# A three-stage kernel on one Trainium2 core: output columns split at row 64, small steps moved between engines

## The reference, cut to what matters

```python
scores = q @ k.T / 8; causal mask; a = exp(scores - rowmax)
a /= a.sum(-1) + 1e-9;  local = a @ v
q_p = where(q > 0, q, exp(q) - 1) + 1                  # "phi"
mem_out = (q_p @ M_prev) / (q_p @ z_prev + 1e-6)
x = g * mem_out + (1 - g) * local                      # g = sigmoid(beta) per head
x = act(x @ w_in) @ w_out                              # 512 -> 2048 -> 512
out = capacity-limited top-1 experts over x, 8 experts 512 -> 1024 -> 512
```

## Time and profile before

| | |
|---|---|
| runs | 307.69 us median (306.95 to 309.27, 3 runs) |
| the profiled execution | 307.44 us, its span 305.3 us |
| busy | PE 98%, DVE 71%, ACT 50%, POOL 45% |
| granted TensorE clock | 1.000, full speed throughout |
| prologue / rounds 1 to 7 / round 8 | 0 to 14.43 / 14.43 to 98.77 / 98.77 to 111.71 us |

### The profile page before, as it was taken

The page is one execution under the profiler, slowest core; times in us unless marked ns, Lnnn a source line. Parts: engine busy times, 40 slices in busy tenths (PEclk is TensorE's granted clock), DMA queues, the critical chain, the costliest instruction groups (busy, mean ns, idle before and its releaser), DMA issues.

```text
span 305.3 us, 7256 instructions
## 1 busy us (share of the span) xinstructions
PE 297.8 (98%) x2821; PEld 247.5 (81%) x2821; DVE 217.4 (71%) x583; ACT 151.4 (50%) x332; POOL 136.4 (45%) x154
## 2 busy tenths in 40 slices
PE   7999999999999999999999999999999999999993
PEld 6666676676666988887999998999989898996863
DVE  3999998999978367897885557955785559880520
ACT  1796866867766244655551444345344546501110
POOL 4878997998998300373782003003312334020031
PEclk9999999999999999999999999999999999999999
DMA  8999798861537700000000407751015019349980
GB/s 164 158 207 228 191 203 174 192 172 46 166 68 206 228 5 0 2 2 0 2 0 2 77 2 287 266 90 30 0 20 93 7 18 384 150 124 392 354 320 9
DMA packets 75047, 38.48 MB, mean 126 GB/s; under 512 B 66008, under 2 KB 66016, under 8 KB 73988
## 3 DMA queue, kind: packets, MB, share of 16 engines
q1 hardware_dynamic: 72340, 36.74, 45.8%
q10 hardware_dynamic: 2416, 0.59, 1.0%
q0 software_dynamic: 256, 0.67, 0.6%
HBM read 32.66 MB, written 5.39 MB: 125 GB/s over the span
## 4 chain that ended last, share of the span: by engine, by line
PE 94%; POOL 2%; DVE 1%; issue 1%; ACT 0%; POOLq 0%
PE bank_a L1841 17%; PE bank_b L1841 17%; PE bank_out L1798 6%; PE bank_a L1697 4%; PE bank_b L1901 4%; PE bank_pt L1901 4%; PE bank_pt L1749 4%; PE bank_a L1775 3%; PE bank_out L1795 2%; PE bank_a L2080 2%; PE bank_out L1874 2%; PE bank_b L2080 2%; PE bank_b L1692 2%; PE bank_out L2189 2%; PE bank_out L1786 2%; PE bank_a L2090 2%
## 5 line engine op out<-in xcount | busy, mean ns | idle before, releaser
L720 POOL TENSOR_SCALAR prob<-prob,rl,gate_loc 128x512 f32<-128x512 f32 (+3 forms) x64 | 41.5, 662 | 11.0 <-DVE rl L1230 11.0
L1841 PE MATMUL bank_a<-x_hi,win_hi 128*128 128x288 f32 x128 | 39.3, 307 | 0.0
L1841 PE MATMUL bank_b<-x_hi,win_hi 128*128 128x288 f32 x128 | 38.2, 298 | 0.0
L1841 PE MATMUL bank_b<-x_lo,win_hi 128*128 128x288 f32 x128 | 38.0, 297 | 0.0
L1841 PE MATMUL bank_b<-x_hi,win_lo 128*128 128x288 f32 x128 | 38.0, 297 | 0.0
L1841 PE MATMUL bank_a<-x_hi,win_lo 128*128 128x288 f32 x128 | 38.0, 297 | 0.0
L1841 PE MATMUL bank_a<-x_lo,win_hi 128*128 128x288 f32 x128 | 37.9, 296 | 0.0
L972 ACT ACTIVATE g_raw<-bank_a,biases 128x576 f32<-128x576 f32 x16 | 11.9, 742 | 49.5 <-DVE sq L1310 49.5
L909 ACT ACTIVATE prob<-prob,negmax 128x512 f32<-128x512 f32 (+3 forms) x64 | 35.0, 549 | 0.3 <-DVE negmax L1180 0.3
L804 POOL TENSOR_TENSOR w_lo<-w_sb,w_hi 128x512 fp32r<-128x512 f32 x8 | 11.4, 1426 | 48.2 <-ACT w_hi L1015 48.2
L749 POOL TENSOR_TENSOR x_lo<-xT,x_hi 128x1152 fp32r<-128x1152 f32 x4 | 10.6, 2662 | 48.6 <-ACT x_hi L922 48.6
(11 more groups left out here) (322 smaller groups left out, 792.2 us busy)
## 6 DMA issues: line engine op xcount, KB each, us to landing
w_sb<-in_moe_w_dram SPq DMA_DIRECT2D x6, 2048.0 KB, 12.0
win_raw<-in_moe_w_in_dram SPq DMA_DIRECT2D x4, 1024.0 KB, 5.6
wout<-in_moe_w_out_dram SPq DMA_DIRECT2D x4, 1024.0 KB, 6.1
win_raw<-in_moe_w_in_dram SPq DMA_DIRECT2D x1, 4096.0 KB, 13.6
out_dram<-zero_row SPq DMA_DIRECT2D x8, 288.0 KB
x_d<-x_rows SPq DMA_DIRECT2D x32, 72.0 KB, 2.1
v_sb<-in_v_dram SPq DMA_DIRECT2D x16, 128.0 KB, 2.5
qn<-in_q_dram SPq DMA_DIRECT2D x24, 72.0 KB, 5.4
```

The lines of the kernel that those rows point to most:

```text
L720: pool.tensor_scalar(prob[u][:, h, :], prob[u][:, h, :], rl[:, c:c + 1], gate_loc[:, 2 * j + h:2 * j + h + 1], ALU.mult, ALU.mult).then_in ...
L1841: last = pe.matmul(h_bank(d)[:, t, :], w[:, m, f:f + P], x[c % 2][:, m, :], start=(m == 0 and n == 0), stop=(m == KT - 1 and n == 2))
```

## The change

1. The tokens now begin at column 448 of `bank_out`: 64 in the first bank, 512 in the second. The memory term is cut the same way, a tile of 64 first, then four of 128. All products of a pair with v stand in one function, six per head with 192, 320, 448, 64, 64 and 512 columns, in place of nine.
2. TensorE's order behind `turn_prob(j, 6)` becomes `add_memory(j)`, `memory(r)`, `values(j)`; `values` waits for copies 2, 5 and 6 before its first product.
3. ScalarE adds the 1e-9 (`row_sums`, behind `exp_s(r, 2)` and `below_zero(r + 1)`, and behind `exp_s(r, 4)`); VectorE keeps the reciprocal alone.
4. Pair 1's q and k are loaded in blocks and turned by VectorE, behind `row_max(0, 4)`; TensorE's ten transposes and VectorE's three copies go. Loads of pair 3 wait for these buffers.
5. From round 2 on, `turn_k(r + 1)` moves from the start of VectorE's round to behind `row_max(r, 4)`; in round 0 `row_factor(0, 1)` stands ahead of `scale_memory(0)`.
6. `few_hidden` goes behind f = 4.

```diff
+        X_AT = NFULL * P - TAIL
+        def mem_tile(t):
+            at = max(0, TAIL + (t - 1) * P)
+            return at, P if t else TAIL
...
-                if n > 3:
+                if n > 2:
                     sp.wait_ge(s_qe, n - 1)
...
-            load_tiles(sp, q_rows[1], q3[2:4, :, :], s_qrow[1])
+            load_blocks(sp, qn[1], q3[2:4, :, :], s_q[1])
...
+            def row_sums(i, part):
+                cols = slice(0, 4) if part == 0 else slice(4, 9)
+                act.wait_ge(s_exp, 5 * i + (2 if part == 0 else 5))
+                act.activation(rl[:, cols], rsum[:, cols], ACT.Identity, bias=biases[:, 2:3]).then_inc(s_eps, 1)
...
             def row_factor(i, part):
                 cols = slice(0, 4) if part == 0 else slice(4, 9)
-                dve.wait_ge(s_exp, 5 * i + (2 if part == 0 else 5))
-                dve.tensor_scalar(rl[:, cols], rsum[:, cols], 1e-9, None, ALU.add).then_inc(s_rl, 1)
-                dve.wait_ge(s_rl, 4 * i + 2 * part + 1)
+                dve.wait_ge(s_eps, 2 * i + part + 1)
                 dve.reciprocal(rl[:, cols], rl[:, cols]).then_inc(s_rl, 1)
...
-            copy_q(1)
-            copy_k(1)
             dve.wait_ge(s_tail, 3)
             row_max(0, 4)
+            turn_q(1)
+            turn_k(1)
+            row_factor(0, 1)
             scale_memory(0)
...
-                    turn_k(r + 1)
-                if r == 1:
-                    row_factor(0, 1)
...
                     row_max(r, 4)
+                if 1 < r < NPAIR - 1:
+                    turn_k(r + 1)
...
-                for c in reversed(range(NFULL)):
-                    times_v(j, c, False)
-            def last_values(j):
                 copied(j, 6)
-                for c in range(NT):
-                    last = times_v(j, c, True)
+                for c, q0, q1 in ((3, 3 * P, S), (2, 2 * P, S), (1, P, S), (NFULL, NFULL * P, S), (0, 0, TAIL), (0, TAIL, S)):
+                    w = P if c < NFULL else TAIL
+                    for h in range(2):
+                        last = pe.matmul(bank_out[D * h:D * h + D, X_AT + q0:X_AT + q1], v_sb[j % 2][0:w, c, h, :],
+                                         probT[0:w, h, c * KSTEP + q0:c * KSTEP + q1], start=False, stop=(c == 0))
...
+                if r == 0:
+                    memory(0)
                 if r > 0:
-                    values(j)
+                    add_memory(j)
                 if 0 < r < NPAIR:
                     memory(r)
-                if r == 0:
-                    turn_k(1)
-                    memory(0)
                 if r > 0:
-                    last_values(j)
+                    values(j)
...
-                if f == 5:
+                if f == 4:
                     few_hidden()
```

More of the change, by code:

```diff
@@ L125, in build_program @@
         mem = [sb(f"mem{p}", [P, NT, 2, D], F32)[0] for p in range(2)]
-        q_rows = [sb(f"q_rows{p}", [P, NT, 2, D], F32, at=xT_at + 4 * NT * P * p)[0] for p in range(2)]
-        k_rows = [sb(f"k_rows{p}", [P, NT, 2, D], F32, at=xT_at + 4 * NT * P * (2 + p))[0] for p in range(2)]
-        assert 16 * NT * P <= 4 * NPAIR * S
+        q_rows, _, _ = sb("q_rows", [P, NT, 2, D], F32, at=xT_at)
+        k_rows, _, _ = sb("k_rows", [P, NT, 2, D], F32, at=xT_at + 4 * NT * P)
+        assert 8 * NT * P <= 4 * NPAIR * S
         maskw, _, _ = sb("maskw", [P, NFULL * P], F32)
@@ L286, in build_program @@
         s_k = [sem(f"s_k{p}") for p in range(2)]
-        s_qrow = [sem(f"s_qrow{p}") for p in range(2)]
-        s_krow = [sem(f"s_krow{p}") for p in range(2)]
+        s_qrow = sem("s_qrow")
+        s_krow = sem("s_krow")
         s_qt = sem("s_qt")
@@ L307, in build_program @@
         s_exp = sem("s_exp")
+        s_eps = sem("s_eps")
         s_rl = sem("s_rl")
@@ L1708, in turn_rows, with turn_q, turn_k @@
                 return last
[L1710 to L1726, removed]
+            def turn_q():
+                pe.wait_ge(s_qrow, 48)
+                turn_rows(bank_b, q_rows, range(NT)).then_inc(s_qt, 1)
+            def turn_k():
+                pe.wait_ge(s_krow, 48)
+                turn_rows(bank_out, k_rows, range(NT)).then_inc(s_kt, 1)
             def spread_beta():
@@ L1742, in turn_prob @@
                 if j == 0 and g == 0:
-                    pe.wait_ge(s_qe, 2)
+                    pe.wait_ge(s_zc, 1)
+                if j == 0 and g == 1:
+                    pe.wait_ge(s_gates, 1)
                 copied(j - (g < 2), (g - 2) % NPT)
@@ L1772, in memory @@
                 for t in range(NT):
+                    at, w = mem_tile(t)
                     for h in range(2):
                         part = slice(D * h, D * h + D)
-                        last = pe.matmul(mem_bank(i)[0:rows[t], t, h, :], qpT[i % 2][part, t * P:t * P + rows[t]], mz[part, i, :],
-                                         start=True, stop=True)
+                        last = pe.matmul(mem_bank(i)[0:w, t, h, :], qpT[i % 2][part, at:at + w], mz[part, i, :], start=True, stop=True)
                 last.then_inc(s_nm, 1)
@@ L1784, in add_memory @@
                 for t in range(NT):
[L1785 to L1795, removed]
-                                         probT[0:w, h, c * KSTEP + NFULL * P:c * KSTEP + S], start=False, stop=(c == NFULL))
-                    else:
-                        last = pe.matmul(bank_t[part, c * P:NFULL * P], v_sb[j % 2][:, c, h, :],
-                                         probT[:, h, c * KSTEP + c * P:c * KSTEP + NFULL * P], start=False, stop=(c == 0))
-                return last
+                    at, w = mem_tile(t)
+                    pe.matmul(bank_out[:, X_AT + at:X_AT + at + w], mem[j % 2][0:w, t, :, :].rearrange("p h d -> p (h d)"),
+                              ident[0:w, 0:w], is_transpose=True, start=(t < 2), stop=False)
             def values(j):
                 pe.wait_ge(s_v[j % 2], 48 * (j // 2 + 1))
-                add_memory(j)
                 copied(j, 2)
                 copied(j, 5)
-                for c in reversed(range(NFULL)):
-                    times_v(j, c, False)
-            def last_values(j):
                 copied(j, 6)
-                for c in range(NT):
-                    last = times_v(j, c, True)
+                for c, q0, q1 in ((3, 3 * P, S), (2, 2 * P, S), (1, P, S), (NFULL, NFULL * P, S), (0, 0, TAIL), (0, TAIL, S)):
[3 more added lines that the diff above has]
+                                         probT[0:w, h, c * KSTEP + q0:c * KSTEP + q1], start=False, stop=(c == 0))
                 last.then_inc(s_pv, 1)
@@ L1964, in keep_running @@
                 for i in range(n):
-                    at = (NT + i % 2) * P
+                    at = S + i % 2 * P
                     pe.transpose(bank_out[:, at:at + P], ident[:, :], ident[:, :])
             keep_running(18)
-            turn_k(0)
-            turn_q(0)
+            turn_k()
+            turn_q()
             spread_beta()
```

76 lines of the change are left out of this document (39 added, 37 removed).

## The result

The changed kernel takes 310.62 us (median of 7 runs, 309.85 to 311.2) against 307.69 us (7 runs, 306.81 to 309.27): ratio 1.0094, 95% interval 1.0074 to 1.0113. On a second chip it took 310.47 us (4 runs) against 308.21 us: 1.0074 (1.0049 to 1.0099). The forecast was 310.0 us and its sum +2.4 us; measured are +2.9 and +2.3 us. The profiled execution took 310.62 us, 3.2 us more than the one before. Its span is 308.8 us instead of 305.3, 3.5 us more; what lies outside the span went from 2.1 to 1.8 us.

A forecast was written before the change was run, and what follows sets the result against it. TensorE was taken to bound the kernel, holding 94% of the chain that ended last. Terms +1.0, +1.4, +0.2, 0, 0 and -0.2 sum to +2.4 us on 307.44; forecast 310.0 us, range 306.8 to 312.0.

The forecast's parts named there:

- The output split: TensorE's six products a head for nine: one more shape change, +0.10 us a round, +0.27 in round 8, sum +1.0.
- Rival A: The output split pays: new shape changes cost nothing, -2.4 us in place of +1.0, 306.6 us; chance 0.13.
- Memory ahead of values in round 1: TensorE in round 1 waits at memory(1) for phi(1), behind ScalarE's sum and the reciprocal: +1.4 us, bounds +0.9 and +1.6.
- Rival D: Round 1 doesn't wait, because VectorE's and ScalarE's work shifts with TensorE's: 308.6 us; chance 0.12.
- Values behind copy 6: First values product waits for copy 6: no wait in rounds 2 to 5 and 7, +0.2 us in round 6.
- The 1e-9 on ScalarE: Addition off VectorE, where GpSimd's subtraction held it and copy 6 would come late by 0.4 us; by itself worth 0.
- Rival B: Reciprocal or ScalarE's sum late, so values wait for copy 6: 0.4 us in six rounds, 312.4 us; chance 0.12.
- Pair 1 by VectorE: Prologue and round 1: earlier memory(0) and GpSimd factors against a later row maximum; sum 0, bounds -0.2 and +0.5 us.
- Rival C: Pair 1's blocks land late, at 14.6 us instead of under 13.4: +1.2 us, 311.2 us; chance 0.08.
- Left tokens: Last stage: few_hidden a step forward removes TensorE's wait for g_fewT, -0.2 us, bounds -0.6 and 0.

The follow-up runs named there:

- e3: Changed kernel with memory tiles in order 1, 2, 3, 4, 0 and the 64-row key tile first among the values, four shape changes instead of eight: 308.07 us.
- e6: Kernel before, nine products a head kept, but memory ahead of all of them and the tail's 64-row key tile first among the values: 309.00 us, ratio 1.0024.
- e1: Changed kernel with phi(1) ahead of row_factor(1, 0) on VectorE in round 1, nothing else: 309.78 us, ratio 1.0044.
- e2: Changed kernel with the 1e-9 added by VectorE again and ScalarE's row_sums calls removed: 310.35 us, ratio 1.0065.
- e5: Changed kernel with e1 and e3 joined, turn_q(2) and below_zero(2) behind phi(1), and row_sums(r, 0) ahead of below_zero every round: 306.50 us, ratio 0.9952.
- e4: Changed kernel with pair 1's q and k loaded as rows again, turned by TensorE and copied by VectorE: 310.71 us, ratio 1.0070.
- e7: Changed kernel with few_hidden back behind f = 5: 310.66 us in one run.

## Why the prediction held, point by point

**The output split.** Said: +0.10 us a round, as one change of shape more less 0.03 for shorter products, and +0.27 in round 8. Measured: +0.12 and +0.29. Both halves were then measured alone: 0.095 a change (e3 against the changed kernel), not 0.12 to 0.15, and 0.03 for the split (e6 against e3). From these the sum would be +0.07. The other 0.05 comes of changes that don't all cost the same: the four that e3 takes from the new order give 0.38, the three that e6 takes from the old one 0.23, so the one change more is worth 0.15, and less 0.03 that is +0.12. The mechanism is shown; that +0.10 came so near is partly luck, since the flat price of 0.12 to 0.15 lies above both averages measured here (0.095 and 0.077). Rival A (new changes cost nothing, 306.6 us) fell: rounds got longer, not under 11.9.

**Memory ahead of values in round 1.** Said +1.4, by a chain through `below_zero(2)`, the addition, the reciprocal and phi. The chain is in the trace just so, a wait of 1.33 us, and e1 takes 0.48 of it away by moving phi alone. The sum was right, its two parts less so: with the addition back on VectorE (e2) the wait is still 1.12 us, where 0.9 was said, because VectorE gets there 0.2 us later in the round than before, and round 1 is only 0.12 shorter, where ScalarE's sum was to cost 0.5. Rival D (no wait, 308.6 us) fell.

**Values behind copy 6.** Said 0 in rounds 2 to 5 and 7, and +0.2 in round 6. Measured: no wait, and 0.2 (`memory` to values 1.50 us instead of 1.30, 85.34 to 86.84 in the trace). e5 shows that ScalarE's order makes it.

**The 1e-9 on ScalarE.** Worth about 0 by itself as said (e2: -0.12, -0.08 and +0.25 in three rounds), but one step of the working was wrong: that the held addition "would now be late by 0.4 us in five rounds". I left GpSimd's subtraction at its old place in the round, though `memory` ahead of the values lets it start earlier (by 0.8 us in e2; by 1.3 in the changed kernel, where it starts at 56.20 in the round from 53.47). With the addition back on VectorE (e2) TensorE waits 0.17 in one round. Rival B (312.4 us) needed a reciprocal held as the addition was. In round 4 VectorE reaches it only as the subtraction ends, but in round 7 of the changed kernel it starts 0.68 us before that end, and is not held:

```profile
93.48 4.55 POOL L752 TENSOR_TENSOR win_lo<-win_raw,win_hi 128x2048 fp32r<-128x2048 f32 x1
...
97.35 0.17 DVE L1245 RECIPROCAL rl<-rl 128x4 f32<-128x4 f32 x1
```

In e5 it starts 1.36 us before the end in round 7 (93.58 against 94.94) and takes 0.17 us too, where the addition of e6, begun 1.46 us before the end, took 1.48. So rival B fell by its own condition, and not only because no wait showed. It was also priced with six rounds, while the subtraction runs in four (2, 4, 5 and 7).

**Pair 1 by VectorE.** Said 0 (bounds -0.2 and +0.5): -0.16 ahead of round 1, and within it a wait of 0.30 for the row maximum against 0.36 got back where GpSimd's factors come earlier. Undone alone (e4), the prologue is 0.3 longer. Rival C (blocks late) fell.

**Left tokens.** Said -0.2. Measured: from the end of round 8 to the product of the left tokens 172.20 us instead of 172.51, -0.31 (-0.16 to the end of the span, because of the unexplained gaps in between). Undone alone (e7), +0.3.

**What the sum did not have.** The first profile's late clock, +1.15 us, is in no term. Nor are the 0.3 us saved outside the span (2.1 to 1.8), whose cause no run shows. With the terms as measured, +2.3, they make the +3.2 of the two profiles. In the medians of two chips the kernel is 2.3 and 2.9 us slower; how much of that the clock's start has, the medians don't tell. The prediction is right by its terms, within 0.1 us of their sum, and not through these two.

## What to carry to other kernels

Count the changes of tile shape before you count products: here four fewer, had by order alone, gave 0.38 us a round, and six products for nine gave 0.03. A step pulled forward on the engine that bounds the kernel meets its producers earlier; read, in the first and the odd rounds too, when each of them is done, and reorder these as well (the wait of 1.33 us in round 1 is 0.64 in e5, by the order of four small steps). And when a step moves, move with it everything that it releases on other engines, before you price a collision between them.

## What the runs showed of the hardware

- Equal 128x128 transposes at the start were 0.21 us apart and later 0.11, although the granted clock is given as 1.00 for both; the switch came between 5.05 and 7.95 us over ten traces of nearly the same start, and moved the first scores by up to 1.3 us (7.48 to 8.80).
- A change of tile shape costs TensorE about 0.1 us (0.38 us for four, 0.23 for three), the products being the same on both sides of each comparison.
- VectorE's small addition, begun in the last 1.5 us of GpSimd's 4.55 us subtraction, ends when that ends (0.23 to 1.48 us instead of 0.16, in rounds of before, e2 and e6).
- VectorE's reciprocal of the same 4 columns, begun beside the same subtraction, is not held: 0.17 us, begun 0.68 us (changed kernel) and 1.36 us (e5) before its end.
- ScalarE does the same addition on 4 columns in 0.28 to 0.30 us.
